# A gated linear attention with two feed-forward stages on one core: split weights kept in DRAM, solver steps and the chain placed anew

## The chip, the cores and the metric

The kernel runs on 1 of the 8 cores of a Trainium2 chip. The metric is the device time of the program in microseconds (us), the median of the timed runs. The profile is of one execution more, with its own time.

## The reference, cut to what matters

```
# attention: B, H, S, D = 4, 8, 768, 48; delta rule, one state (D x D) for each batch and head
k_n = k / (norm(k) + 1e-6)
for t in range(S):
    y[t] = q[t] @ state
    state = state + beta[t] * outer(k_n[t], v[t] - k_n[t] @ state)
x = y, as 3072 tokens x 384
x = (x @ w_a) * (x @ w_b) @ w_out                  # d_ff 1536
h = x @ w_in                                       # d_ff 2048
out = (max(h, 0) + alpha * min(h, 0)) @ w_out2
```

All is float32. The kernel keeps the precision of the big products by splitting every operand into a high and a low part in the 32-bit matmul format fp32r (hi, and lo = raw - hi) and summing three matmuls: hi*hi, hi*lo, lo*hi.

## The kernel before, in words

**Tiles and units.** The 768 steps are cut into 12 chunks of 64 (T) steps, and two chunks (a pair) of all four batches make one tile of 512 tokens, six tiles (NP) in all. In a tile the two feed-forward stages run as 68 units (NU, `tile_units`, L197). A unit is one 128 x 384 piece of a weight against the tile: A f and BB f (x times w_a and w_b, 9 matmuls of 512 columns each), O f (times w_out, 9 of 512), H f (times w_in, 9 of 512) and Y f (times the second w_out, 12 of 384). The order is A0, BB0, then A f, BB f, O f-1 for f = 1 to 11 (so BB f is unit 3f, O f is unit 3f+4), O11 as unit 35 (`last_o`), H0, H1, then H f, Y f-2, and Y14, Y15. The number m = 68 i + n names unit n of tile i.

**The order of all work** is one list, `seq`, written by hand (L169 to L262). Every engine walks through this list and does its own part of each entry, in order. Beside each unit of tile i, the lists of `beside(i + 1)` (L211) hang the attention work of the next pair: transposes (TR) and Gram products (GG, DG), a solver that inverts a 32 x 32 triangular block for every head and half on VectorE (IN, 34 steps ROW 1 to 34, XT; `solver`, L724), and the chain (H1, H2, H3, H4, HS, HY for each of the two chunks, L160), in which TensorE makes small matmuls and ScalarE or VectorE evacuates them before the next stage can start. VS (L937, GpSimd) scales v by the key norms. Before the first tile a prologue does all this for pair 0 and parts of pair 1, with idle time of TensorE filled by throw-away matmuls F (L450).

Where `beside` puts things before: ROW 1 to 14 four per unit from unit 11, ROW 15 to 18 at units 15 to 18, ROW 19 to 34 one per unit at units 19 to 34; XT and VS of the first chunk at unit 35, VS of the second at 36; H1 at 35, then H2 at 38 and one chain stage at every unit up to HY of the second chunk at 48; the reload of x (XL) at 50; norms of the next pair at 51 to 54. Loads of k, q for the pair after (LTK, LTQ) stand at units 8 to 15, LK at 17 and 19.

**Weights.** There is a ring of 9 slots (RG). WL n (L343, SyncE's queue) waits until the unit that used the slot 9 units ago is done and loads 192 KB into `w_raw`: O and Y as rows of 1536 B, A, BB and H as rows of 512 B. WS n stands 4 units (RS) ahead of unit n: ScalarE casts `w_raw` to `w_hi` (L669) and GpSimd subtracts to `w_lo` (L952), which lies in the memory of `w_raw`. TensorE waits for `lo_ok` before each unit. So each of the 408 pieces is loaded and split anew in each of the six tiles.

**Within a unit.** For BB f, VectorE makes g_sb from e_sb and the bank (L895), ScalarE casts it to g_hi (L691), VectorE subtracts to g_lo (L906, entry GL, which stands behind all that `beside` hangs on that unit), and O f needs g_lo. For H f, ScalarE makes e_sb and f_sb (L687, L688), VectorE g_sb (L900), then g_hi and g_lo as above. After O11 the three banks are evacuated to m_hi, m_lo (M, L698, L911) for H0.

In the chain, H1 is evacuated by VectorE, which waits for VS of its chunk:

```
                    dve.wait_ge(*is_full(*st))
                    dve.wait_ge(v_ok, c + 1)
                    dve.tensor_tensor(r_sb[:, hf], v_raw[:, c % 2, units(hf), :], chained(hf), ALU.subtract
```

and H2 on TensorE waits for XT:

```
                        pe.wait_ge(solve, NSOL * p + NSOL)
```

Of the kernel before, what the change touches and what calls it, by code (L numbers as in the profile page):

```python
# [8 lines left out]
F32 = mybir.dt.float32  # L9
# [5 lines left out]
def build(nc, q, k, v, beta, wa, wb, wo, win, wout, alpha, out):  # L15
# [25 lines left out]
    assert 2 * T == P and 2 * U == SB and TILE == 512  # L41

    ctx = ExitStack()
    with ctx:
# [21 lines left out]
        with ExitStack() as whole:  # L66
            w_raw = sb("w_raw", [P, RG, DM], F32, whole)
            x_raw = sb("x_raw", [P, KC, TILE], F32, whole)
            g_sb = sb("g_sb", [P, GR, TILE], F32, whole)
        w_lo = sb("w_lo", [P, RG, DM], F32R)  # L70
        x_lo = sb("x_lo", [P, KC, TILE], F32R)
        g_lo = sb("g_lo", [P, GR, TILE], F32R)
        w_hi = sb("w_hi", [P, RG, DM], F32R)
        x_hi = sb("x_hi", [P, KC, TILE], F32R)
# [95 lines left out]
        seq += [("LV", 0), ("LV", 1), ("B",)] + [("F", 0)] * 4 + flat(norms(0))  # L170
        for hf in range(2):
            seq += [("TRK", 2 * hf)] + [("F", 0)] * 3 + [("TRK", 2 * hf + 1)] + [("F", 0)] * 2
            seq += [("GK", 0, hf), ("GK", 1, hf), ("DG0", hf)]
        seq += [("IN", 0)]
        for b in range(B):
            seq += [("LTK", 1, b), ("LTQ", 1, b)]
        seq += [("LK", 1, 0), ("LK", 1, 1)] + [("WL", n) for n in range(RG)] + [("VS", 0), ("VS", 1)]
        for n in range(1, ROWS + 1):
# [3 lines left out]
                    21: [("GQ", 1, 0)], 22: [("GQ", 1, 1)]}.get(n, [])  # L182
        seq += [("XT", 0), ("F", ROWS), ("F", ROWS)]
        beside0 = {(0, "H2"): [("PT", 0), ("PT", 1), ("SQ", 2)], (0, "H3"): [("PT", 2), ("PT", 3), ("KS", 2), ("SQ", 3)],
                   (0, "H4"): [("KS", 3), ("KN", 1)], (0, "HS"): [("KI", 1), ("LV", 2)], (0, "HY"): [("XL", 0, 0, T)],
                   (1, "H1"): [("WS", 0)], (1, "H2"): [("WS", 1)], (1, "H3"): [("WS", 2)], (1, "H4"): [("WS", 3)]}

        for kind in ("H2", "H3", "H4", "HS", "HY"):
            seq += both(kind, 0) + [("F", 0)] + beside0.get((0, kind), [])
        for kind in ("H1", "H2", "H3", "H4", "HY", "HS"):  # L190
# [20 lines left out]
        def beside(p):  # L211
            at = [[] for _ in range(NU)]
            if p >= NP:
                return at
            if p > 1:
                for g in range(8):
                    at[g // 2].append(("TR", p, g))
                for g in range(4):
                    at[4 + g // 2].append(("GG", 2 * p, g))
                    at[6 + g // 2].append(("GG", 2 * p + 1, g))  # L220
                for j in range(2):
                    at[6 + j].append(("DG", 2 * p, j))
                    at[8 + j].append(("DG", 2 * p + 1, j))

            s = 10
            at[s].append(("IN", p))
            for n in range(1, ROWS + 1):
                at[s + ((n + 3) // 4 if n <= R8 else 4 + n - R8 if n <= R16 else 8 + n - R16)].append(("ROW", p, n))
            at[s + 8 + ROWS - R16 + 1] += [("XT", p), ("VS", 2 * p)]
            at[s + 8 + ROWS - R16 + 2].append(("VS", 2 * p + 1))  # L230

            s += 8 + ROWS - R16 + 3
            for n, st in enumerate(chain(2 * p) + chain(2 * p + 1)):
                m = s + n // 2 if n >= 2 else last_o
                at[m].append(st)
                if p + 1 < NP and st[0] == "H2" and st[2] == 0:
                    at[m].append(("LV", st[1] + 2))
            s += len(chain(0)) + 1
            at[s].append(("XL", p, 0, P))
            if p + 1 < NP:  # L240
                for b in range(B):
                    at[8 + 2 * b].append(("LTK", p + 1, b))
                    at[9 + 2 * b].append(("LTQ", p + 1, b))
                for j in range(2):
                    at[17 + 2 * j].append(("LK", p + 1, j))
                for j, part in enumerate(norms(p + 1)):
                    at[s + 1 + j] += part
            return at

        for i in range(NP):  # L250
            for n, (st, extra) in enumerate(zip(tile_units(i), beside(i + 1))):
                m = NU * i + n
                seq += [st] + [("WL", m + RG)] * (m + RG < NU * NP) + [("WS", m + RS)] * (m + RS < NU * NP)
                if st[0] == "O" and st[2] == NF1 - 1:
                    seq += [("M", i, kc) for kc in range(KC)]
                seq += extra
                if st[0] in ("BB", "H"):
                    seq.append(("GL", i, st[2] + NF1 * (st[0] == "H")))
# [49 lines left out]
        def _(sp):  # L308
            for st in seq:
# [33 lines left out]
                elif kind == "WL":  # L343
# [38 lines left out]
        def _(pe):  # L382
            def three(dst, lhs_hi, lhs_lo, rhs_hi, rhs_lo, start, stop):
                pe.matmul(dst, lhs_hi, rhs_hi, start=start, stop=False)  # L384
                pe.matmul(dst, lhs_hi, rhs_lo, start=False, stop=False)  # L385
                return pe.matmul(dst, lhs_lo, rhs_hi, start=False, stop=stop)  # L386

            def in_bank(*st):
# [6 lines left out]
            for st in seq:  # L395
# [126 lines left out]
                elif kind in ("A", "BB"):  # L522
# [18 lines left out]
                elif kind == "O":  # L541
# [16 lines left out]
                elif kind == "H":  # L558
# [417 lines left out]
```

## Time and profile before

| what | us |
|---|---|
| median of 3 timed runs (1168.53 to 1175.56) | 1168.88 |
| the profiled execution, whole time | 1172.99 |
| its span, first to last instruction | 1171.3 |

In the views, PE is TensorE (matmuls), PEld its weight loads, DVE VectorE, ACT ScalarE, POOL GpSimd, SP SyncE with its DMA queue. In brackets behind a row of the order of time stands how long the engine sat idle before it, and what released it. Matmuls are pipelined: one 128x512 matmul is shown with 0.39 us but the next starts 0.227 us after it, so durations of units are read from the start of one to the start of the next. Granted clock 1.00 is the upper of TensorE's two levels (2.4 GHz), 0.50 the lower (1.2 GHz).

The view of busy time by stretch has these columns: the stretch (us from the span's start) and its length, then busy us (and number of instructions) of PE, PEld, DVE, ACT and POOL, the granted clock, the mean busy share of the 16 DMA engines and the GB/s that they moved.

### The profile page before, as it was taken

To read this page: it belongs to the slowest core of one execution; us is meant where nothing else is said; L and a number is where in the kernel's file an instruction comes from. 1 tells how busy PE (TensorE), PEld (TensorE's weight loads), DVE (VectorE), ACT (ScalarE), POOL (GpSimd) and SP (SyncE) were. 2 spreads that over 40 slices of the span, in tenths; PEclk is the share of its full clock that TensorE was granted. 3 is DMA by queue.
4 is the path that set the end of the run, shared out by engine and by line. 5 is a ranking of instruction groups with operands and counts; after the bars stand their busy time and mean duration, and the time that the engine had idled before them with its cause. 6 is when DMAs were issued, how large, how long until landed. Compare 5 with 4: busy or idle time off the path is not lost.

```text
span 1171.3 us, 24961 instructions
## 1 busy us (share of the span) xinstructions
PE 1122.2 (96%) x10390; PEld 948.6 (81%) x10390; DVE 585.2 (50%) x849; ACT 530.4 (45%) x1054; POOL 477.7 (41%) x432
## 2 busy tenths in 40 slices
PE   5899999999998999999999999899999999999998
PEld 3587877898886889887789888689888778988898
DVE  5834774334577334387424377533348733422333
ACT  2134343365434356543436554345644334644564
POOL 0012562245364225255224446423536522555453
PEclk9889998999999999999899999899999989999999
DMA  9721732233452234272224354223323212443331
GB/s 118 150 43 50 180 90 62 64 108 108 116 135 81 57 89 122 69 168 82 63 59 121 99 136 122 68 63 102 115 63 101 75 43 61 117 122 98 92 95 61
DMA packets 235919, 110.26 MB, mean 94 GB/s; under 512 B 111376, under 2 KB 235808, under 8 KB 235808
## 3 DMA queue, kind: packets, MB, share of 16 engines
q1 hardware_dynamic: 235776, 108.66, 36.3%
q8 instruction: 83, 1.36, 0.5%
q14 instruction: 28, 0.23, 0.1%
q0 software_dynamic: 32, 0.01, 0.0%
HBM read 99.20 MB, written 4.72 MB: 89 GB/s over the span
## 4 chain that ended last, share of the span: by engine, by line
PE 87%; DVE 7%; ACT 3%; issue 1%; DMA 0%; SPq 0%; POOL 0%; DVEq 0%; POOLq 0%
PE bank L384 24%; PE bank L385 23%; PE bank L386 23%; PE bank L447 3%; PE bank L463 2%; PE bank L484 2%; PE bank L520 2%; PE bank L519 2%; PE bank L497 2%; PE bank L487 2%; DVE g_sb L900 2%; PE bank L404 1%; DVE x_lo L884 1%; DVE prod L782 1%; PE bank L481 1%
## 5 line engine op out<-in xcount | busy, mean ns | idle before, releaser
L952 POOL TENSOR_TENSOR w_lo<-w_raw,w_hi 128x384 fp32r<-128x384 f32 x408 | 457.6, 1135 | 637.2 <-ACT w_hi L669 636.3
L691 ACT CAST g_hi<-g_sb 128x512 fp32r<-128x512 f32 x168 | 104.2, 620 | 242.9 <-DVE g_sb L895 144.8
L669 ACT CAST w_hi<-w_raw 128x384 fp32r<-128x384 f32 x408 | 196.9, 511 | 0.3
L900 DVE SCALAR_TENSOR_TENSOR g_sb<-f_sb,neg_alpha,e_sb 128x512 f32<-128x512 f32 x96 | 82.2, 857 | 210.7 <-ACT f_sb L688 205.4
L384 PE MATMUL bank<-x_hi,w_hi 128*128 128x512 f32 x432 | 172.0, 398 | 3.0 <-DVE x_lo L884 2.6
L385 PE MATMUL bank<-x_lo,w_hi 128*128 128x512 f32 x432 | 169.1, 391 | 0.0
L386 PE MATMUL bank<-x_hi,w_lo 128*128 128x512 f32 x432 | 168.8, 391 | 0.0
L906 DVE TENSOR_TENSOR g_lo<-g_sb,g_hi 128x512 fp32r<-128x512 f32 x168 | 120.5, 717 | 74.3 <-ACT g_hi L691 72.7
L687 ACT ACTIVATE e_sb<-bank 128x512 f32<-128x512 f32 x96 | 57.2, 596 | 170.5 <-PE bank L386 170.5
L384 PE MATMUL bank<-w_hi,g_hi 128*128 128x384 f32 x384 | 132.1, 344 | 0.0
L386 PE MATMUL bank<-w_hi,g_lo 128*128 128x384 f32 x384 | 129.2, 337 | 0.0
L385 PE MATMUL bank<-w_lo,g_hi 128*128 128x384 f32 x384 | 128.8, 335 | 0.0
L895 DVE TENSOR_TENSOR g_sb<-e_sb,bank 128x512 f32<-128x512 f32 x72 | 49.4, 686 | 154.5 <-PE bank L386 154.5
L384 PE MATMUL bank<-m_hi,w_hi 128*128 128x512 f32 x288 | 119.0, 413 | 0.1
L385 PE MATMUL bank<-m_lo,w_hi 128*128 128x512 f32 x288 | 116.4, 404 | 0.0
L386 PE MATMUL bank<-m_hi,w_lo 128*128 128x512 f32 x288 | 116.1, 403 | 0.0
L384 PEld LDWEIGHTS bank<-x_hi,w_hi 128*128 128x128 f32 x432 | 81.4, 188 | 23.1 <-DVE x_lo L884 4.9
L384 PE MATMUL bank<-g_hi,w_hi 128*128 128x512 f32 x216 | 87.5, 405 | 11.5 <-DVE g_lo L906 11.5
L680 ACT COPY e_sb<-bank 128x512 f32<-128x512 f32 x72 | 42.3, 587 | 124.0 <-PE bank L386 123.6
L386 PEld LDWEIGHTS bank<-x_hi,w_lo 128*128 128x128 f32 x432 | 81.5, 189 | 17.2
L385 PEld LDWEIGHTS bank<-x_lo,w_hi 128*128 128x128 f32 x432 | 81.6, 189 | 16.1
L385 PE MATMUL bank<-g_lo,w_hi 128*128 128x512 f32 x216 | 87.0, 403 | 0.0
(105 smaller groups left out, 1714.0 us busy)
## 6 DMA issues: line engine op xcount, KB each, us to landing
w_raw<-in_moe_w_out_dram SPq DMA_DIRECT2D x168, 192.0 KB, 2.4
w_raw<-in_moe_w_in_dram SPq DMA_DIRECT2D x96, 192.0 KB, 2.4
w_raw<-in_moe_w_a_dram SPq DMA_DIRECT2D x72, 192.0 KB, 2.5
w_raw<-in_moe_w_b_dram SPq DMA_DIRECT2D x72, 192.0 KB, 2.6
k_raw<-in_k_dram SPq DMA_DIRECT2D x24, 192.0 KB, 4.1
k_tok<-in_k_dram SPq DMA_DIRECT2D x24, 192.0 KB, 3.4
q_tok<-in_q_dram SPq DMA_DIRECT2D x24, 192.0 KB, 3.4
v_raw<-in_v_dram SPq DMA_DIRECT2D x24, 192.0 KB, 3.9
```

What stands on the lines that cost most here:

```text
L384: pe.matmul(dst, lhs_hi, rhs_hi, start=start, stop=False)
L385: pe.matmul(dst, lhs_hi, rhs_lo, start=False, stop=False)
L386: return pe.matmul(dst, lhs_lo, rhs_hi, start=False, stop=stop)
L447: mm = pe.matmul(bk[h, 2 * T * j:2 * T * (j + 1)], kq[rows, w, e, 0], kq[rows, w, e].rearrange("p i t -> p (i t)"), start=True, stop=True)
L669: act.copy(w_hi[:, n % RG], w_raw[:, n % RG]).then_inc(hi_ok, 1)
L680: act.copy(e_sb[:, f % 2], h_bank[0][:, :]).then_inc(e_ok, 1)
L687: act.activation(e_sb[:, f % 2], h_bank[f % 2][:, :], ACT.Relu).then_inc(e_ok, 1)
L691: act.copy(g_hi[:, j % GR], g_sb[:, j % GR]).then_inc(gh_ok, 1)
L895: dve.tensor_tensor(g_sb[:, j % GR], e_sb[:, f % 2], h_bank[1][:, :], ALU.mult).then_inc(g_ok, 1)
L900: dve.scalar_tensor_tensor(g_sb[:, j % GR], f_sb[:, f % 2], neg_alpha[:, f:f + 1], e_sb[:, f % 2], ALU.mult, ALU.add).then_inc(g_ok, 1)
L906: dve.tensor_tensor(g_lo[:, s], g_sb[:, s], g_hi[:, s].bitcast(F32), ALU.subtract).then_inc(gl_ok, 1)
L952: pool.tensor_tensor(w_lo[:, r], w_raw[:, r], w_hi[:, r].bitcast(F32), ALU.subtract).then_inc(lo_ok, 1)
```

## The change

1. A DRAM scratch tensor of 68 x 128 x 768 floats is added. `w_hi` and `w_lo` of a slot now lie side by side in one tensor `w_two`. In the first tile each unit's split pair, 384 KB in rows of 3072 B, is stored to it (new entry WT, on SyncE's queue). From the second tile on, WL loads that pair straight into `w_two`; WS isn't done there, and TensorE waits for the load itself (`weights`).
2. The solver's steps stand at other units: ROW 1 to 14 seven per unit at 11 and 12, ROW 15 to 18 at 13 to 16, ROW 19 to 34 at 17 to 28 by the list `r16`; XT and the first VS at 29, the second VS at 31.
3. The chain stands at units 28, 30, 31, 32, 33, 34 (first chunk) and 35, 37, 39, 41, 43, 45 (second chunk); XL at 46, the norms at 47 to 50.
4. In the prologue, the second half's transposes stand ahead of the first half's block copies, four more F follow XT, and two F instead of one stand behind each of the five chain stages of chunk 0.

```diff
+    split = nc.dram_tensor("split_scratch", (NU, P, 2 * DM), F32).ap()
...
-            w_raw = sb("w_raw", [P, RG, DM], F32, whole)
+            w_ring = sb("w_ring", [P, RG, 2, DM], F32, whole)
...
-        w_lo = sb("w_lo", [P, RG, DM], F32R)
+        w_raw = w_ring[:, :, 1]
+        w_two = sb("w_two", [P, RG, 2, DM], F32R)
+        w_hi, w_lo = w_two[:, :, 0], w_two[:, :, 1]
...
-        for hf in range(2):
-            seq += [("TRK", 2 * hf)] + [("F", 0)] * 3 + [("TRK", 2 * hf + 1)] + [("F", 0)] * 2
-            seq += [("GK", 0, hf), ("GK", 1, hf), ("DG0", hf)]
-        seq += [("IN", 0)]
+        seq += [("TRK", 0)] + [("F", 0)] * 3 + [("TRK", 1)] + [("F", 0)] * 2 + [("GK", 0, 0), ("GK", 1, 0)]
+        seq += [("TRK", 2)] + [("F", 0)] * 3 + [("TRK", 3)] + [("DG0", 0), ("GK", 0, 1), ("GK", 1, 1), ("DG0", 1), ("IN", 0)]
...
-        seq += [("XT", 0), ("F", ROWS), ("F", ROWS)]
+        seq += [("XT", 0)] + [("F", ROWS)] * 6
...
-                   (1, "H1"): [("WS", 0)], (1, "H2"): [("WS", 1)], (1, "H3"): [("WS", 2)], (1, "H4"): [("WS", 3)]}
+                   (1, "H1"): [("WS", 0)], (1, "H2"): [("WS", 1)], (1, "H3"): [("WS", 2)], (1, "H4"): [("WS", 3)],
+                   (1, "HY"): [("WT", 0), ("WT", 1)], (1, "HS"): [("WT", 2)]}
...
-            seq += both(kind, 0) + [("F", 0)] + beside0.get((0, kind), [])
+            seq += both(kind, 0) + [("F", 0)] * 2 + beside0.get((0, kind), [])
...
             for n in range(1, ROWS + 1):
-                at[s + ((n + 3) // 4 if n <= R8 else 4 + n - R8 if n <= R16 else 8 + n - R16)].append(("ROW", p, n))
-            at[s + 8 + ROWS - R16 + 1] += [("XT", p), ("VS", 2 * p)]
-            at[s + 8 + ROWS - R16 + 2].append(("VS", 2 * p + 1))
-
-            s += 8 + ROWS - R16 + 3
+                r16 = (7, 8, 9, 9, 10, 10, 11, 11, 11, 12, 13, 14, 15, 16, 17, 18)
+                at[s + ((n + 6) // 7 if n <= R8 else 2 + n - R8 if n <= R16 else r16[n - R16 - 1])].append(("ROW", p, n))
+            at[s + 19] += [("XT", p), ("VS", 2 * p)]
+            at[s + 21].append(("VS", 2 * p + 1))
+
+            stages = (28, 30, 31, 32, 33, 34, last_o, last_o + 2, last_o + 4, last_o + 6, last_o + 8, last_o + 10)
             for n, st in enumerate(chain(2 * p) + chain(2 * p + 1)):
-                m = s + n // 2 if n >= 2 else last_o
+                m = stages[n // 2]
...
-            s += len(chain(0)) + 1
+            s = stages[-1]
+            s += 1
             at[s].append(("XL", p, 0, P))
...
-                seq += [st] + [("WL", m + RG)] * (m + RG < NU * NP) + [("WS", m + RS)] * (m + RS < NU * NP)
+                seq += [st] + [("WL", m + RG)] * (m + RG < NU * NP) + [("WS", m + RS)] * (m + RS < NU)
+                seq += [("WT", m + RS - 1)] * (m + RS - 1 < NU)
...
                     if n >= RG:
                         sp.wait_ge(unit_ok, n - RG + 1)
-                    if which in ("O", "Y"):
+                        if n - RG < NU:
+
+                            sp.wait_ge(w_st[n % RG], 16 * ((n - RG) // RG + 1))
+                    if n >= NU:
+                        sp.dma_start(w_two[:, n % RG].bitcast(F32).rearrange("p i c -> p (i c)"), split[u]).then_inc(w_ld[n % RG], 16)
+                    elif which in ("O", "Y"):
...
+                elif kind == "WT":
+                    n = st[1]
+                    sp.wait_ge(lo_ok, n + 1)
+                    sp.dma_start(split[n], w_two[:, n % RG].bitcast(F32).rearrange("p i c -> p (i c)")).then_inc(w_st[n % RG], 16)
...
+            def weights(n):
+                if n < NU:
+                    pe.wait_ge(lo_ok, n + 1)
+                else:
+                    pe.wait_ge(w_ld[n % RG], 16 * (n // RG) + 16)
...
-                    pe.wait_ge(lo_ok, n + 1)
+                    weights(n)
```

The last replacement is made in all four kinds of unit (A and BB, O, H, Y).

## Rows read from the trace of the kernel before

**Rows 1.** Busy time by stretch: prologue, tiles 0, 1, 2, last tile.

```profile
0.00:97.70 97.70, 77.75 (x1310) 56.31 (x1310) 58.44 (x105) 29.27 (x56) 9.69 (x18) 0.90 0.58 94
97.70:275.50 177.80, 172.68 (x1556) 147.81 (x1556) 90.69 (x124) 79.46 (x160) 78.32 (x69) 0.96 0.38 98
275.50:462.70 187.20, 182.09 (x1716) 155.11 (x1716) 98.51 (x143) 88.06 (x175) 80.46 (x71) 0.98 0.37 98
462.70:651.00 188.30, 183.17 (x1716) 156.52 (x1716) 98.50 (x143) 88.06 (x175) 80.45 (x71) 0.97 0.37 97
...
1026.50:1171.30 144.80, 141.25 (x660) 121.22 (x660) 45.04 (x64) 70.97 (x142) 68.17 (x66) 1.00 0.31 93
```

**Rows 2.** Waits of PE, whole span: us in total, times, longest.

```profile
PE bank L484 <- ACT w_sb L652: 14.2, 5, 2.9
PE bank L384 <- DVE g_lo L906: 11.5, 6, 2.2
```

**Rows 3.** PE in order of time, tile 1: start, us, engine, line, operation.

```profile
340.88 0.39 PE L384 MATMUL bank<-x_hi,w_hi 128*128 128x512 f32 x1
...
342.92 0.39 PE L384 MATMUL bank<-x_hi,w_hi 128*128 128x512 f32 x1
...
361.63 0.49 PE L384 MATMUL bank<-g_hi,w_hi 128*128 128x512 f32 x1 [2.23 <-DVE g_lo L906]
...
365.44 2.07 PE L463 MATMUL bank<-state,kq 48*64 48x48 f32 x64
...
380.46 1.55 PE L484 MATMUL bank<-w_sb,gs 32*32 32x48 f32 x64 [2.80 <-ACT w_sb L652]
...
385.68 1.60 PE L487 MATMUL bank<-r_sb,xt 32*32 32x48 f32 x64
...
407.55 1.55 PE L484 MATMUL bank<-w_sb,gs 32*32 32x48 f32 x64
...
411.26 1.55 PE L487 MATMUL bank<-r_sb,xt 32*32 32x48 f32 x64
```

**Rows 4.** DVE in order of time, tile 1, around the two stalls.

```profile
358.10 2.02 DVE L782 TENSOR_TENSOR prod<-inv,mid 128x1024 f32<-128x1024 f32 x1
...
366.77 2.14 DVE L789 STREAM_TRANSPOSE xt<-inv 128x1024 f32<-128x1024 f32 x1
368.80 0.98 DVE L857 TENSOR_TENSOR r_sb<-v_raw,bank 128x384 f32<-128x384 f32 x2
...
373.99 2.05 DVE L900 SCALAR_TENSOR_TENSOR g_sb<-f_sb,neg_alpha,e_sb 128x512 f32<-128x512 f32 x1 [0.80 <-PE bank L386]
...
378.21 0.75 DVE L900 SCALAR_TENSOR_TENSOR g_sb<-f_sb,neg_alpha,e_sb 128x512 f32<-128x512 f32 x1 [0.80 <-ACT f_sb L688]
```

**Rows 5.** POOL and ACT in order of time, tile 1, second stall.

```profile
374.02 1.47 POOL L945 TENSOR_TENSOR v_raw<-v_raw,knorm 128x768 f32<-128x768 f32 x1
...
379.94 0.85 ACT L652 COPY w_sb<-bank 128x384 f32<-128x384 f32 x2
```

**Rows 6.** ACT and POOL behind an A unit, tile 0.

```profile
118.01 0.59 ACT L680 COPY e_sb<-bank 128x512 f32<-128x512 f32 x1 [1.84 <-PE bank L386]
118.50 0.52 ACT L669 CAST w_hi<-w_raw 128x384 fp32r<-128x384 f32 x1
...
119.09 1.01 POOL L952 TENSOR_TENSOR w_lo<-w_raw,w_hi 128x384 fp32r<-128x384 f32 x1 [1.18 <-ACT w_hi L669]
```

**Rows 7.** Busy time by stretch: loads of k and q, of weights.

```profile
12.50:15.00 2.50, 2.50 (x48) 1.60 (x48) 1.01 (x5) 1.01 (x2) 0.00 (x0) 1.00 1.51 164
...
50.00:52.50 2.50, 1.71 (x6) 0.42 (x4) 2.47 (x2) 0.00 (x0) 1.51 (x2) 0.77 1.05 313
```

**Rows 8.** DMA issues: count, KB each, median us to landing.

```profile
w_raw<-in_moe_w_out_dram SPq DMA_DIRECT2D x168, 192.0 KB, 2.4
```

**Rows 9.** PE in the prologue: H3 of chunk 0 and of chunk 1.

```profile
56.19 2.77 PE L484 MATMUL bank<-w_sb,gs 32*32 32x48 f32 x64
...
71.92 1.55 PE L484 MATMUL bank<-w_sb,gs 32*32 32x48 f32 x64
```

More of the change, by code:

```diff
@@ L66, in build @@
         with ExitStack() as whole:
-            w_raw = sb("w_raw", [P, RG, DM], F32, whole)
+            w_ring = sb("w_ring", [P, RG, 2, DM], F32, whole)
             x_raw = sb("x_raw", [P, KC, TILE], F32, whole)
             g_sb = sb("g_sb", [P, GR, TILE], F32, whole)
-        w_lo = sb("w_lo", [P, RG, DM], F32R)
+        w_raw = w_ring[:, :, 1]
+        w_two = sb("w_two", [P, RG, 2, DM], F32R)
+        w_hi, w_lo = w_two[:, :, 0], w_two[:, :, 1]
         x_lo = sb("x_lo", [P, KC, TILE], F32R)
         g_lo = sb("g_lo", [P, GR, TILE], F32R)
-        w_hi = sb("w_hi", [P, RG, DM], F32R)
         x_hi = sb("x_hi", [P, KC, TILE], F32R)
@@ L123, in build @@
         dg_ok, dgv_ok, solve = sem("dg_ok"), sem("dgv_ok"), sem("solve")
-        w_ld = [sem(f"w_ld{n}") for n in range(RG)]
+        w_ld, w_st = [sem(f"w_ld{n}") for n in range(RG)], [sem(f"w_st{n}") for n in range(RG)]
         hi_ok, lo_ok, unit_ok = sem("hi_ok"), sem("lo_ok"), sem("unit_ok")
@@ L547, in _ @@
                         pe.wait_ge(od_ok, 2 * i)
-                    pe.wait_ge(lo_ok, n + 1)
+                    weights(n)
                     pe.wait_ge(gl_ok, NF * i + f + 1)
@@ L566, in _ @@
                         pe.wait_ge(f_ok, NF2 * i + f - 1)
-                    pe.wait_ge(lo_ok, n + 1)
+                    weights(n)
                     for kc in range(KC):
@@ L578, in _ @@
                     r = n % RG
-                    pe.wait_ge(lo_ok, n + 1)
+                    weights(n)
                     pe.wait_ge(gl_ok, NF * i + NF1 + f + 1)
```

## Prediction, made before the changed kernel was run

> **What bounds the kernel now.** I read the busy times by stretch first, then TensorE's waits, then the order of time of each engine around the waits. TensorE is busy in 97% of a middle tile (182.1 of 187.2 us), VectorE, ScalarE and GpSimd in about half of it [rows 1]. So only what stops TensorE or slows it counts. Its pace elsewhere is fixed: a unit of 9 matmuls takes 342.92 - 340.88 = 2.04 us [rows 3], and the last tile, with no attention beside it, takes 144.8 us for its 68 units [rows 1].
>
> Two waits make up nearly all idle time of TensorE behind the prologue, each once in each of the five tiles that carry attention: g_lo 2.2 us before O11, and w_sb 2.8 us before H3 [rows 2]. After each, TensorE is slow for a few us more: O11 takes 365.44 - 361.63 = 3.81 us, where a unit with a chain stage behind it takes some 2.2; H3 and the unit behind it take 385.68 - 380.46 = 5.22, while the same pair one chunk later takes 411.26 - 407.55 = 3.71 [rows 3]. A stall thus costs its idle time and a slow stretch: 2.23 + 1.6 = 3.8 us, and 2.80 + 1.5 = 4.3 us, 8.1 us a tile. Every second tile is 1.1 us longer with the same busy instructions (188.3 against 187.2) [rows 1], which I read as a longer slow stretch: 9.2 us there.
>
> Why they arise: the first, because VectorE runs a solver product of 2.02 us between g_sb and g_lo of BB11 [rows 4], and O11 follows BB11 by one unit only. The second, because g_sb of an H unit takes 2.05 us instead of 0.75 [rows 4], from the same moment on which GpSimd runs VS (374.02, 1.47 us) [rows 5]; ScalarE gets to w_sb only behind that unit's and the next one's casts.
>
> **The change part by part, against the profiled execution (1172.99 us; its span 1171.3; it lies 4.1 us above the median of the runs).**
>
> *Solver and chain moved, tiles 1 to 4.* No solver step stands at BB11 (unit 33) any more; HY stands at unit 34 between it and O11, 2 times about 1.9 us of matmuls, so g_lo has 5.8 us, of which it needs some 3 (g_sb, the HS evacuation, g_lo). The first stall goes whole. H3 of chunk 2 stands at unit 31 behind H2 at 30: on ScalarE g_hi and two w_sb copies (0.85) [rows 5] against one unit of 2.04; it fits. H3 of the next chunk has two units behind H2, and VS is gone from there: GpSimd has nothing else to do from tile 1 on, so it does VS for the next pair as soon as the norms are there, near unit 50, where H f and Y f have five units between them. The second stall goes whole. What is late next? XT must be there at H2, behind unit 30. Counted from the end of BB9 (unit 27): VectorE does g_sb, a solver step of 1.9, g_lo, one of 1.2 (4.4 us), two H1 evacuations (0.98) and XT (2.14) [rows 4]: 7.6 us. TensorE does O8, H1, A10, BB10: 2.1 + 2.0 + 2.2 + 2.1 = 8.4. It fits by 0.8 us. M at unit 35 keeps H1 as its cover. Sum: 8.1 x 2 + 9.2 x 2 = -34.6 us.
>
> *The same in tile 0.* Its two stalls go, -9.2. But here the solution of pair 1 needs VS, and GpSimd's queue has WS of unit 33 ahead of it, whose cast stands on ScalarE behind the copy of A10 (unit 29). VectorE's H1 at unit 28 waits for this VS and holds XT behind it, and TensorE's H2 waits for XT. From the end of A10: e_sb and cast 1.0, w_lo to 2.1 [rows 6], VS 1.47 [rows 5] to 3.6, two evacuations to 4.6, XT to 6.7 [rows 4]. TensorE has only BB10 (2.1): idle 4.6 us, and by the two stalls above a slow stretch of 1.5 to 4, taken as 2.5. +7.1. Tiles 1 to 4 have no WS, so this is tile 0's alone. Net -2.1.
>
> *Weights loaded split.* ScalarE loses 340 casts of 0.51, GpSimd 340 subtractions of about 1 us [rows 5, 6]: neither ends a wait other than those two, so nothing more comes back; the rest was cover. In tiles 1 to 5 SyncE issues one load a unit as before, 384 KB instead of 192, 9 units ahead (18 us; a load of today lands in 2.4 [rows 8]) and no longer 4 units ahead of a cast. The wait on w_st asks for a store issued three units before, also nothing. No row shows 3 KB rows moving. Rates that rows do show: 313 GB/s while weights are loaded, 164 GB/s while k and q come in 192 B rows [rows 7]. So 384 KB take 1.26 or 2.4 us; were the packets the whole cost, a third of a 192 KB load's 0.63, 0.2 us. I take 1.26, the row with the longest runs. At 1.26 tiles 1 to 5 have room (1.26 of 2.04 us).
>
> *Stores in tile 0.* From unit 0 to 19: 20 loads x 0.63 + 20 stores x 1.26 + 12 loads of k and q x 1.2 = 52.2 us of DMA beside 42.6 us of TensorE: 9.6 us behind. A load is issued 5 units (10.2) ahead of its cast and lands in 2.4, so 7.8 are free; ScalarE and then TensorE wait 1.8 us. With 0.2 us a store: nothing; with 2.4: see below. I put +1. SyncE itself issues at most three DMAs of 0.4 us a unit; behind a WT that waits for lo_ok it holds the next WL, four units early, so nothing.
> By the Trainium skill's "SBUF — State Buffer", section "A bandwidth-pool intuition that's wrong (but worth ruling out)", a core gets about 358 GB/s of HBM; a store would then take an estimated 1.10 us, the queue be 6.4 us behind, and this term 0 instead of 1. The 313 GB/s of the row lie below that figure; no row reaches down to decide it.
>
> *Prologue (97.7 us).* The reordered copies take one of two ScalarE block copies off the path to the solver, about -1. Four more F fall into XT's 2 us. Five more F cost 0.3 to 0.54 each (+2), and if they bring the upper clock back sooner, each stage of chunk 0 wins up to 2.77 - 1.55 = 1.2 us [rows 9] (-5 at most). I take -1 in all, between +2 and -5. Loads of the first weights have over 20 us.
>
> *Against the removal of GpSimd's work:* with subtractions still running in tile 0, VectorE keeps being held there as in rows 4. In "SBUF — State Buffer", section "SBUF: two separate sides", the Trainium skill calls the port that VectorE and GpSimd share an exclusive lock for the whole instruction. Row and rule agree on the 2.05 us; by it the 0.8 us of room before XT would go only in tile 0, where that wait is lost already.
>
> Sum: -34.6 - 2.1 + 1 - 1 = -36.7. Profiled 1136.3 us; on the scale of the median 1168.9 - 36.7 = **1132 us**.
>
> **The rivals.**
> 1. *DMA sets tile 0* (chance 0.13). For it: stores double what the queue carries and k, q, v come on top. Against: rows 7's 313 GB/s were reached with a third of the run length. At 1.6 us a store the early part is 52.2 + 6.8 = 59 us, 16.4 behind, 8.6 us of stall instead of 1, with its slow stretch +9: 1141. Sign: queue share near 1 over tile 0.
> 2. *The moved solver is late in every tile* (0.10): 0.8 us of room before XT turns into a wait, by queueing I can't see. About 1 us idle and 2 slow, four tiles: +12, 1144. The change then does two thirds of what it says.
> 3. *Tile 0 doesn't stall at v* (0.12), or the F bring the clock back: -7, 1125. Against it stands the order of the queues alone.
> 4. *Slower than before* (0.03): 3 KB rows move no faster than the 192 B rows, 2.4 us for 384 KB. Then 68 loads take 163 us a tile, plus 16 attention loads x 1.2 = 19: 182 against a clean tile of 179 (187.2 - 8.1): +3 x 4; the last tile 163 instead of 142, +21; tile 0 68 x 3.03 + 19 = 225 instead of 176, +49. 1132 + 82 = 1214. It decides from about 2.35 us a load in tiles 1 to 4, 2.1 in the last one.
>
> **How the numbers follow.** Forecast 0.62 (own range 1126 to 1139, from the prologue's ends and the slow stretch), rivals 0.13, 0.10, 0.12, 0.03. The range takes in rivals 1 to 3 and the few us by which executions differ: 1119 to 1146. A measurement of this kernel tells 1% (12 us) from no change: faster by more in all cases but the fourth and unknown ones, 0.94; within 1% 0.03; slower 0.03.
>
> **What would show it.** Right: a middle tile of 179 us in the busy times by stretch, the waits for g_lo and w_sb gone from TensorE's list in tiles 0 to 4, GpSimd busy only in the first quarter of the span, DMA at 130 to 160 GB/s from tile 1 on. In tile 0 one new wait of 4 to 5 us before H2 at unit 30, released by XT. Wrong: a TensorE wait on a split_scratch load, VectorE's XT ending after BB10 in tiles 1 to 4, a tile 0 longer than 180 us.

## The result and the profile after

The changed kernel takes 1132.04 us (median of 4 runs, 1130.89 to 1133.91) against 1170.03 us before (4 runs); the ratio is 0.967, with a 95% interval of 0.963 to 0.970. The forecast was 1132 us. The profiled execution took 1133.91 us with a span of 1132.2, 39.1 us less than before.

Busy time by stretch of the changed kernel, in the columns of [rows 1]: prologue, tiles 0, 1, 2 and the last one, cut at the first matmul of each.

```profile
0.00:95.23 95.23, 75.11 (x1318) 52.88 (x1318) 58.25 (x105) 29.19 (x56) 9.68 (x18) 0.96 0.63 109
95.23:273.34 178.11, 173.12 (x1557) 147.80 (x1557) 90.73 (x124) 78.01 (x157) 80.14 (x68) 0.96 0.76 248
273.34:452.03 178.69, 178.69 (x1717) 153.48 (x1717) 89.27 (x143) 60.16 (x107) 3.79 (x2) 1.00 0.62 178
452.03:630.60 178.57, 178.57 (x1718) 153.38 (x1718) 88.63 (x142) 60.17 (x107) 3.79 (x2) 1.00 0.61 178
987.73:1132.20 144.47, 141.00 (x661) 121.15 (x660) 43.03 (x62) 44.78 (x78) 0.00 (x0) 1.00 0.56 176
```

In tiles 1 and 2 TensorE's busy time now equals the stretch, at a granted clock of 1.00, the upper level (2.4 GHz); before it was 182 of 187 us at 0.98 [rows 1]. Each of tiles 1 to 4 is 178.6 us long, the alternation of 187 and 188 is gone. GpSimd has two instructions a tile left, the DMA moves 178 GB/s instead of 98. Tile 0 is as long as before, 178.1 us against 177.8. The prologue is 2.5 us shorter, the last tile 0.3. Executions of the kernel before differ by 7 us (1168.53 to 1175.56), and the profiled one lies above their median, so the difference of the profiles (39.1) is a little larger than that of the medians (38.0).

TensorE's waits over the whole span, to be held against [rows 2] (us in total, times, longest; line numbers are those of the changed kernel: L502 is H2, L399 a big matmul):

```profile
PE bank L502 <- DVE xt L810: 4.7, 1, 4.7
...
PE bank L399 <- DVE x_lo L905: 2.6, 1, 2.6
...
PE bank L399 <- DVE g_lo L927: 0.6, 2, 0.3
```

The w_sb wait of 14.2 us is gone, that for g_lo fell from 11.5 to 0.6, and one new wait has come, in tile 0. VectorE in order of time around it, then GpSimd and TensorE:

```profile
158.99 1.47 DVE L927 TENSOR_TENSOR g_lo<-g_sb,g_hi 128x512 fp32r<-128x512 f32 x1
160.38 1.21 DVE L807 TENSOR_REDUCE inv<-prod 128x64 f32<-128x1024 f32 x1
165.97 1.02 DVE L878 TENSOR_TENSOR r_sb<-v_raw,bank 128x384 f32<-128x384 f32 x2 [4.37 <-POOL v_raw L966]
166.90 2.00 DVE L810 STREAM_TRANSPOSE xt<-inv 128x1024 f32<-128x1024 f32 x1
```

```profile
163.42 1.01 POOL L973 TENSOR_TENSOR w_two<-w_ring,w_two 128x384 fp32r<-128x384 f32 x1 [2.08 <-ACT w_two L690]
164.39 1.47 POOL L966 TENSOR_TENSOR v_raw<-v_raw,knorm 128x768 f32<-128x768 f32 x1
```

```profile
169.01 2.36 PE L502 MATMUL bank<-r_sb,xt 32*32 32x48 f32 x64 [4.66 <-DVE xt L810]
```

This is the chain of waits that was forecast: the subtraction behind the cast of unit 33, then VS, then the H1 evacuations, which were free to run 4.37 us earlier, then XT, then H2.

One engine's rows show something else, VectorE's product of 128x768 in tile 0 and, with nothing on GpSimd, in tile 1:

```profile
153.12 2.37 DVE L803 TENSOR_TENSOR prod<-inv,mid 128x768 f32<-128x768 f32 x1
...
338.88 1.61 DVE L803 TENSOR_TENSOR prod<-inv,mid 128x768 f32<-128x768 f32 x1
```

### The profile page after: what moved, and what is told of

The parts are those of the page before. It is cut to its first block, busy times and chain, and to the rows that moved or that the text cites. A ratio compares the mean times of both kernels' runs of the same rounds, so it can differ in the third digit from the quotient of the medians.

```text
span 1132.2 us, 24435 instructions
## 1 busy us (share of the span) xinstructions
PE 1103.6 (97%) x10397; PEld 935.4 (83%) x10397; DVE 544.2 (48%) x849; ACT 390.9 (35%) x714; POOL 101.2 (9%) x92
## 4 chain that ended last, share of the span: by engine, by line
PE 91%; DVE 6%; issue 1%; ACT 1%; POOL 0%; DMA 0%; SPq 0%; DVEq 0%; POOLq 0%
PE bank L399 25%; PE bank L401 24%; PE bank L400 24%; PE bank L468 3%; PE bank L541 2%; PE bank L540 2%; PE bank L484 2%; PE bank L518 2%; PE bank L502 2%; PE bank L505 2%; PE bank L425 1%; PE bank L508 1%; PE bank L475 1%; DVE prod L803 1%; DVE prod L796 1%
## 5 line engine op out<-in xcount | busy, mean ns | idle before, releaser
L399 PE MATMUL bank<-x_hi,w_two 128*128 128x512 f32 x432 | 173.8, 402 | 2.7 <-DVE x_lo L905 2.6
L400 PE MATMUL bank<-x_lo,w_two 128*128 128x512 f32 x432 | 169.7, 393 | 0.0
L401 PE MATMUL bank<-x_hi,w_two 128*128 128x512 f32 x432 | 169.4, 392 | 0.0
L401 PE MATMUL bank<-w_two,g_lo 128*128 128x384 f32 x384 | 129.4, 337 | 0.0
L399 PE MATMUL bank<-w_two,g_hi 128*128 128x384 f32 x384 | 129.3, 337 | 0.0
L400 PE MATMUL bank<-w_two,g_hi 128*128 128x384 f32 x384 | 128.9, 336 | 0.0
L399 PE MATMUL bank<-m_hi,w_two 128*128 128x512 f32 x288 | 115.6, 401 | 0.1
L401 PE MATMUL bank<-m_hi,w_two 128*128 128x512 f32 x288 | 113.5, 394 | 0.0
L400 PE MATMUL bank<-m_lo,w_two 128*128 128x512 f32 x288 | 113.3, 393 | 0.0
L399 PEld LDWEIGHTS bank<-x_hi,w_two 128*128 128x128 f32 x432 | 81.7, 189 | 22.1 <-DVE x_lo L905 3.3
L401 PEld LDWEIGHTS bank<-x_hi,w_two 128*128 128x128 f32 x432 | 81.8, 189 | 17.5
L400 PEld LDWEIGHTS bank<-x_lo,w_two 128*128 128x128 f32 x432 | 81.9, 190 | 15.6
L399 PE MATMUL bank<-g_hi,w_two 128*128 128x512 f32 x216 | 87.6, 406 | 0.6 <-DVE g_lo L927 0.6
L400 PE MATMUL bank<-g_lo,w_two 128*128 128x512 f32 x216 | 85.0, 394 | 0.0
L401 PE MATMUL bank<-g_hi,w_two 128*128 128x512 f32 x216 | 84.8, 393 | 0.0
```

## The experiments

All were timed against the kernel before on the same chip. They come from three chips, so between experiments the ratios say more than the medians. "Tile 1" is the second tile, from its first matmul to the next one's.

### The parts by themselves

**The split weights alone** (e1_weights): the changed kernel with solver, chain and prologue as before.

```diff
...
-            at[s + 19] += [("XT", p), ("VS", 2 * p)]
-            at[s + 21].append(("VS", 2 * p + 1))
...
+            at[s + 8 + ROWS - R16 + 1] += [("XT", p), ("VS", 2 * p)]
+            at[s + 8 + ROWS - R16 + 2].append(("VS", 2 * p + 1))
...
-            stages = (28, 30, 31, 32, 33, 34, last_o, last_o + 2, last_o + 4, last_o + 6, last_o + 8, last_o + 10)
+            s += 8 + ROWS - R16 + 3
...
-                m = stages[n // 2]
+                m = s + n // 2 if n >= 2 else last_o
...
```

> The split weights alone (part 1), with the solver, the chain and the prologue as before. Theory: the w_sb wait goes with GpSimd's and ScalarE's work, the g_lo wait stays, since the solver's product of 1.9 us still stands between g_sb and g_lo of BB11; it is shorter by the 0.75 us for which g_lo itself was held. Tiles 1 to 4 then take 178.6 + 1.5 idle + 1.6 slow = 181.7 us, tile 0 177.8, the span 97.7 + 177.8 + 4 x 181.7 + 144.5 = 1147 us. Rival, the placing does it all: both waits stay, tiles of 187 to 188, span 1171.

Measured: 1142.81 us, ratio 0.977 (0.974 to 0.980), span 1143.1. Tile 1 takes 180.4 us. TensorE's waits in it:

```profile
362.30 0.47 PE L399 MATMUL bank<-g_hi,w_two 128*128 128x512 f32 x1 [1.45 <-DVE g_lo L927]
...
377.03 1.55 PE L505 MATMUL bank<-w_sb,gs 32*32 32x48 f32 x64 [0.30 <-ACT w_sb L673]
```

The w_sb wait is down to 0.30 us with the chain left where it was, the g_lo wait to 1.45, about the 1.5 that were expected. What was not: no slow stretch follows it, and from H3 to H4 it takes 3.72 us. In tile 0, where GpSimd still subtracts, both waits stay (2.2 and 2.9 us). Of the 36.6 us that tiles 1 to 4 gained together, this part alone gives 29 (four tiles of 180.4 against 751.0 us before).

**The new places alone** (e2_places): parts 2 and 3 on the kernel before.

```diff
-                at[s + ((n + 3) // 4 if n <= R8 else 4 + n - R8 if n <= R16 else 8 + n - R16)].append(("ROW", p, n))
-            at[s + 8 + ROWS - R16 + 1] += [("XT", p), ("VS", 2 * p)]
...
+                at[s + ((n + 6) // 7 if n <= R8 else 2 + n - R8 if n <= R16 else r16[n - R16 - 1])].append(("ROW", p, n))
+            at[s + 19] += [("XT", p), ("VS", 2 * p)]
...
```

> The new places of solver and chain alone (parts 2 and 3) on the kernel before. Theory: GpSimd still has a subtraction per unit in every tile, so VS of the first chunk is late in all five tiles as it was in tile 0 of the changed kernel (4.7 us idle and 3.3 slow): tiles of 178 (tile 0) and 178.6 + 8 = 186.6, span 97.7 + 178 + 4 x 186.6 + 144.7 = 1167 us, no gain worth the name. Rival, the two parts add up: the placing alone removes both waits, span 1135.

Measured: 1178.66 us, ratio 1.008 (1.005 to 1.011): slower than before by more than its interval. TensorE's waits:

```profile
PE bank L483 <- DVE xt L791: 23.2, 5, 4.7
PE bank L386 <- DVE g_lo L908: 6.6, 10, 0.9
```

The wait of tile 0 stands in all five tiles, 4.65 us each, and tiles 1 to 4 take 188.6 to 189.9 us. The mechanism was that of the theory; its price was 2 to 3 us a tile too low, for two short g_lo waits a tile and the slow stretches. So with VS at units 29 and 31 the placing is worth something only where GpSimd doesn't subtract: 180.4 - 178.6 = 1.8 us a tile on top of the split weights. Without them it costs 1.4 to 1.7 us a tile (188.6, 189.7, 188.9 and 189.9 against 187.2, 188.3, 187.2 and 188.3).

**The F of the prologue** (e3_old_f).

```diff
-        seq += [("XT", 0)] + [("F", ROWS)] * 6
+        seq += [("XT", 0), ("F", ROWS), ("F", ROWS)]
...
-            seq += both(kind, 0) + [("F", 0)] * 2 + beside0.get((0, kind), [])
+            seq += both(kind, 0) + [("F", 0)] + beside0.get((0, kind), [])
```

> The changed kernel with the F matmuls of before in the prologue (two behind XT, one behind each stage of chunk 0), the reordered copies kept. Theory: the F hold the upper clock, so without them chunk 0 runs at the lower one (stages of 2.7 us) and A0 starts 2.5 us later; the first unit wins 1.2 back: span 1133.5. Rival, the reordered copies won the 2.5 us: span unchanged, 1132.2.

Measured: 1132.88 us, ratio 0.969 (0.966 to 0.971), span 1131.0. The F do hold the clock: H2, H3 and H4 of chunk 0, first in the changed kernel, then without the added F.

```profile
54.01 1.55 PE L502 MATMUL bank<-r_sb,xt 32*32 32x48 f32 x64
56.03 1.55 PE L505 MATMUL bank<-w_sb,gs 32*32 32x48 f32 x64
58.05 1.55 PE L508 MATMUL bank<-r_sb,xt 32*32 32x48 f32 x64
```

```profile
52.18 1.55 PE L502 MATMUL bank<-r_sb,xt 32*32 32x48 f32 x64 [1.01 <-POOL r_sb L966]
53.98 2.24 PE L505 MATMUL bank<-w_sb,gs 32*32 32x48 f32 x64
56.69 2.77 PE L508 MATMUL bank<-r_sb,xt 32*32 32x48 f32 x64
```

But A0 starts at 96.11 against 95.23 us, and by the end of tile 0 the kernel without them is 1.1 us ahead in its profile, because its tile 0 takes 176.1 us and not 178.1. H2 of chunk 0 starts 54.01 - 52.18 = 1.8 us later with them, of which 0.9 had arisen before any added F (the second pair of GK starts at 19.32 against 18.46 us). What the F are worth in all lies below what these runs tell apart: in the profiles of three kernels with the same prologue (the changed one, e4 and e7 below) tile 0 starts at 95.23, 93.93 and 94.11 us. The six profiles with the old prologue (the kernel before, e1, e2, e8, e9, e10) have it at 96.4 to 98.8, 97.8 in the mean, so the new order and the F together are worth some 3 us.

### What made the two waits

**VS alone** (e8_before_vs), on the kernel before.

```diff
-            at[s + 8 + ROWS - R16 + 1] += [("XT", p), ("VS", 2 * p)]
-            at[s + 8 + ROWS - R16 + 2].append(("VS", 2 * p + 1))
+            at[s + 8 + ROWS - R16 + 1].append(("XT", p))
+            at[s + 12].append(("VS", 2 * p))
+            at[s + 13].append(("VS", 2 * p + 1))
```

> The kernel before with nothing moved but VS, from units 35 and 36 to 22 and 23. Theory: g_sb of H1 takes 0.75 us again, so w_sb comes 1.3 us earlier and the wait before H3 falls from 2.8 to 1.5 us in each of five tiles; the g_lo wait stays: span 1171.3 - 6.5 = 1165. Rival, the port isn't what holds g_sb: 1171.

Measured: 1155.06 us, ratio 0.989 (0.986 to 0.992), span 1153.3: 18 us less in the profiles and 13.6 in the medians, instead of 6.5. TensorE at H3 and H4 of tile 1:

```profile
375.19 1.55 PE L485 MATMUL bank<-w_sb,gs 32*32 32x48 f32 x64 [1.52 <-ACT w_sb L653]
...
378.93 1.55 PE L488 MATMUL bank<-r_sb,xt 32*32 32x48 f32 x64
```

The wait is the expected 1.5 us. But from H3 to H4 it is now 3.74 us, not 5.22 [rows 3]: the slow stretch is gone with the last part of the stall, and with it the longer tile in every second place (184.2 to 184.3 us each). A wait of 1.5 us costs 1.5 here, one of 2.8 costs 4.3 and more.

**g_lo ahead of the solver's steps** (e9_gl_first), on the kernel before.

```diff
-                seq += extra
                 if st[0] in ("BB", "H"):
                     seq.append(("GL", i, st[2] + NF1 * (st[0] == "H")))
+                seq += extra
```

> The kernel before with one entry moved in the list: g_lo of a BB or H unit stands ahead of what hangs beside the unit, not behind it. Theory: the solver's product no longer lies between g_sb and g_lo of BB11, so the g_lo wait falls from 2.2 to the bare chain's 0.3 us and its slow stretch goes, 3.8 us in each of five tiles; the w_sb wait stays: span 1171.3 - 19 = 1152. Rival: VectorE now stands idle 0.7 us for g_hi in each BB unit, its solver steps slip past H2's need of XT, and half of it is lost: 1161.

Measured: 1168.13 us, ratio 0.997 (0.996 to 0.999), span 1166.2. Both theories fall. The same two places in tile 1:

```profile
356.28 0.47 PE L384 MATMUL bank<-g_hi,w_hi 128*128 128x512 f32 x1 [0.31 <-DVE g_lo L906]
...
374.20 2.77 PE L484 MATMUL bank<-w_sb,gs 32*32 32x48 f32 x64 [3.21 <-ACT w_sb L652]
...
380.97 1.55 PE L487 MATMUL bank<-r_sb,xt 32*32 32x48 f32 x64
```

The first wait is gone, as expected, and the tile is as long as ever (187.6 us; tiles 2 to 4 take 187.7, 187.8 and 186.9, tile 0 175.2 instead of 177.9). The second wait grew from 2.80 to 3.21, H3 itself now runs at the lower clock (2.77 us), and from H3 to H4 it takes 380.97 - 374.20 = 6.77 us where it took 5.22 [rows 3]. Unit by unit against tile 1 of the kernel before: O10 and O11 with H1 win 1.9 and 1.3 us; the unit in which the w_sb wait and H3 stand loses 1.6, units 20 to 22, where VectorE now stands idle for g_hi, 0.55, and five further places 0.2 to 0.4 each. So a stall of 2.2 us was taken away and its gain given back behind it, half of it in the other stall. Why that one grew by 0.4 us can be read from VectorE:

```profile
361.80 2.22 DVE L789 STREAM_TRANSPOSE xt<-inv 128x1024 f32<-128x1024 f32 x1
363.92 0.96 DVE L857 TENSOR_TENSOR r_sb<-v_raw,bank 128x384 f32<-128x384 f32 x2
364.81 0.73 DVE L900 SCALAR_TENSOR_TENSOR g_sb<-f_sb,neg_alpha,e_sb 128x512 f32<-128x512 f32 x1
```

TensorE now comes earlier to H0, but XT and the H1 evacuations don't, so g_sb of H0 has to wait behind them (before, VectorE stood idle for 1.27 us ahead of it). ScalarE waits 1.31 us for this g_sb instead of 0.92, and w_sb stands behind it in ScalarE's queue.

**Both** (e10_gl_vs): the edit above, and VS at units 4 and 5.

```diff
-            at[s + 8 + ROWS - R16 + 1] += [("XT", p), ("VS", 2 * p)]
-            at[s + 8 + ROWS - R16 + 2].append(("VS", 2 * p + 1))
+            at[s + 8 + ROWS - R16 + 1].append(("XT", p))
+            at[4].append(("VS", 2 * p))
+            at[5].append(("VS", 2 * p + 1))
```

> The kernel before with two moves in the list only: g_lo ahead of what hangs beside its unit, and VS at units 4 and 5. No DRAM scratch, all weights split anew in each tile, solver and chain where they were. Theory: the two waits are all that the change removes, so this comes near it: tiles of 184.2 - 3.8 = 180.4, span 1153.3 - 19 = 1134, against 1132.2 of the changed kernel. Rival: the w_sb wait comes back to its 2.8 us because VectorE's queue shifts: 1145 or more.

Measured: 1156.9 us, ratio 0.987 (0.984 to 0.991), span 1155.3; no better than VS alone. The w_sb wait stays at 9.6 us in five tiles, 1.9 each, again 0.4 us more than without g_lo ahead (1.5 in e8):

```profile
PE bank L485 <- ACT w_sb L653: 9.6, 5, 1.9
```

and four of the five are followed by a slow stretch: from H3 to H4 it takes 5.3 us in tiles 1, 3 and 4, 6.5 in tile 2, but 3.75, the full pace, in tile 0. With VS away, what stands ahead of w_sb on ScalarE is three H units' worth of e, f and g_hi and the casts of the weights between them; e1 took those casts and the subtractions away, and the wait was 0.3. That the casts and not GpSimd's subtractions are the larger share of this last piece was not tried apart.

### Tile 0

**VS earlier in the changed kernel** (e4_vs_early): XT stays at unit 29, VS goes to 22 and 23.

```diff
-            at[s + 19] += [("XT", p), ("VS", 2 * p)]
-            at[s + 21].append(("VS", 2 * p + 1))
+            at[s + 19].append(("XT", p))
+            at[s + 12].append(("VS", 2 * p))
+            at[s + 13].append(("VS", 2 * p + 1))
```

> The changed kernel with VS at units 22 and 23 instead of 29 and 31. Theory: tile 0's only long wait (4.66 us before H2, 3.3 us slow behind it) goes, tile 0 takes 170 us, span 1124.3. Rival 1, tile 0 is held by the DMA queues (share 1.04 in units 18 to 32): the wait goes but others come, span 1129 or more. Rival 2, VectorE, busy 27.6 of 28 us there, is what is late: VS moved into that stretch holds it longer, g_lo waits grow, span 1127.

Measured: 1124.53 us, ratio 0.960 (0.957 to 0.963), span 1122.2. Tile 0 takes 169.4 us and the 4.66 us wait is gone. Of the 8.7 us that the tile is shorter than in the changed kernel's profile, VS gives 5.9: 7.8 are won at H2 and the unit behind it, 1.9 lost around a new wait. The other 2.8 are not its work. They come from the first two units, which stand behind the same wait of 2.65 us for x_lo and run at another granted clock, 0.57 in the changed kernel and 1.00 in e4 (busy time by stretch, one line each):

```profile
95.23:102.24 7.01, 7.01 (x18) 5.55 (x19) 0.00 (x0) 1.80 (x4) 1.01 (x1) 0.57 0.21 75
```

```profile
93.93:98.14 4.21, 4.21 (x18) 3.49 (x19) 0.00 (x0) 1.81 (x4) 0.63 (x1) 1.00 0.11 29
```

The new wait, 1.54 us, stands at O8, in a stretch where GpSimd stood behind VS and VectorE's solver:

```profile
153.44 0.50 PE L400 MATMUL bank<-g_hi,w_two 128*128 128x512 f32 x1 [1.54 <-POOL w_two L974]
```

**Stores doubled** (e7_store_twice), timed once.

```diff
+    again = nc.dram_tensor("again_scratch", (NU, P, 2 * DM), F32).ap()
...
-                            sp.wait_ge(w_st[n % RG], 16 * ((n - RG) // RG + 1))
+                            sp.wait_ge(w_st[n % RG], 32 * ((n - RG) // RG + 1))
...
-                    sp.dma_start(split[n], w_two[:, n % RG].bitcast(F32).rearrange("p i c -> p (i c)")).then_inc(w_st[n % RG], 16)
+                    for to in (split, again):
+                        sp.dma_start(to[n], w_two[:, n % RG].bitcast(F32).rearrange("p i c -> p (i c)")).then_inc(w_st[n % RG], 16)
```

> The changed kernel with each split pair stored twice, to two scratch tensors. It prices a store of 384 KB where nothing but the DMA can be late. Theory, 1.26 us a store at the 313 GB/s of the kernel before: tile 0 has 68 x (0.63 + 2.52) + 19 = 233 us of DMA and becomes as long, 55 us more: span 1187. Rival, 3 KB rows store at 400 GB/s or more (1.0 us): 68 x 2.6 + 19 = 196, span 1150.

Measured: 1151.41 us, span 1149.7, 17.5 us more than the changed kernel, near the rival's number. Busy time by stretch in tile 0, units 18 to about 30 and the ones behind, and 20 us of the latter:

```profile
134.00:162.00 28.00, 23.23 (x110) 17.21 (x110) 17.02 (x22) 6.75 (x13) 8.76 (x9) 1.00 1.06 345
162.00:200.00 38.00, 28.19 (x449) 22.92 (x447) 14.68 (x17) 9.22 (x19) 13.81 (x12) 0.82 1.00 359
164.00:184.00 20.00, 10.60 (x87) 8.55 (x88) 9.30 (x9) 5.70 (x12) 8.63 (x8) 0.72 1.04 388
```

With the queues full the DMA moves 345 and 359 GB/s in the two stretches, so 384 KB (393,216 bytes) cost by estimate 393.2 / 359 = 1.10 us and not 1.26. The Trainium skill gives about 358 GB/s of HBM for a core ("SBUF — State Buffer", section "A bandwidth-pool intuition that's wrong (but worth ruling out)"). The 38 us agree with that figure, but it is no upper bound here: the 20 us inside them show 388 GB/s, which would be 1.01 us for 384 KB. Nor is the rival's price of 1.0 us borne out by the span: over all of tile 0 (195.8 us, where it said 196) the DMA moves 333 GB/s and not 400. TensorE then waits 7.3 us in ten pieces for w_lo, 3.8 us once for g_lo and 8.4 us for XT. In the changed kernel the first of these stretches moves 315 GB/s at a share of 1.03, and no wait of TensorE ends in a load.

### A version that beats both

**XS ahead of the last two GG** (e5_xs_early).

```diff
-        seq += [("TR", 1, g) for g in range(8)] + [("GG", 2, g) for g in range(4)] + [("GG", 3, g) for g in range(4)]
-        seq += [("XS", 0, kc) for kc in range(KC)] + [("DG", c, j) for c in (2, 3) for j in range(2)]
+        seq += [("TR", 1, g) for g in range(8)] + [("GG", 2, g) for g in range(4)] + [("GG", 3, 0), ("GG", 3, 1)]
+        seq += [("XS", 0, kc) for kc in range(KC)] + [("GG", 3, 2), ("GG", 3, 3)] + [("DG", c, j) for c in (2, 3) for j in range(2)]
```

> The changed kernel with the three XS of tile 0 ahead of the last two GG of the prologue, in the list of all work. Theory: x_lo is ready when TensorE ends its last GG, so the 2.65 us before A0 and the slow stretch behind it (1.96 + 0.97) go: span 1132.2 - 5.6 = 1126.6. Rival, VectorE's evacuations, pushed behind x_lo, hold TensorE's last GG instead: no more than 1 us won, span 1131.

Measured: 1129.52 us, ratio 0.964 (0.961 to 0.967), span 1126.9. The wait before A0 falls from 2.65 to 0.62 us. In the profile it is worth 5.3 us where 5.6 were expected, in the medians 2.5, and the interval of the ratio overlaps that of the changed kernel (0.963 to 0.970). The profile flatters it: the first two units, which took 7.0 us in the changed kernel's profile, take 4.5 here, and e4 has them at 4.2 with the wait still there. The 2.0 us of wait are the part that is sure.

**Both moves** (e6_both): the diffs of e4 and e5 together, with VS at 22 and 23.

> Both moves together. Theory: they add up, span 1132.2 - 7.9 - 5.6 = 1118.7. Rival: an earlier start of tile 0 by 5.6 us brings its DMA queue behind (the loads of k, q stand at units 8 to 19), part of it is lost: 1121 or more.

Measured: 1122.07 us, ratio 0.958 (0.954 to 0.961), span 1120.3: 10 us less than the changed kernel in the medians, with the O8 wait of 1.5 us still there. That the DMA takes the rest isn't seen in any wait.

**VS at units 4 and 5** (e11_best), where VectorE has no solver step, and XS moved as in e5:

```diff
-            at[s + 19] += [("XT", p), ("VS", 2 * p)]
-            at[s + 21].append(("VS", 2 * p + 1))
+            at[s + 19].append(("XT", p))
+            at[4].append(("VS", 2 * p))
+            at[5].append(("VS", 2 * p + 1))
```

> The changed kernel with VS at units 4 and 5, where VectorE has nothing to do, instead of 22 and 23, and XS of tile 0 ahead of the last two GG. Theory: the 1.54 us wait for w_lo at unit 28, which VS at 22 and 23 brought by holding GpSimd's queue, goes with its slow stretch of 1.7: span 1120.3 - 3.2 = 1117. Rival: that wait comes from the subtractions held by VectorE's solver steps, with or without VS: 1120.

Measured: 1120.48 us, ratio 0.957 (0.954 to 0.959), span 1118.9, the lowest of all, though its interval overlaps that of e6. Its prologue, tile 0 and tile 1:

```profile
0.00:91.62 91.62, 73.76 (x1317) 52.14 (x1317) 56.98 (x102) 27.52 (x53) 9.68 (x18) 0.96 0.66 113
91.62:260.06 168.44, 167.54 (x1557) 143.29 (x1557) 92.32 (x128) 79.67 (x159) 80.33 (x68) 1.00 0.80 262
260.06:438.73 178.67, 178.67 (x1717) 153.48 (x1717) 89.30 (x143) 60.16 (x107) 3.79 (x2) 1.00 0.64 179
```

The O8 wait is gone, so it was VS in GpSimd's queue that had brought it; tile 0 won 1.4 us over e6, half of what was expected. The whole of tile 0 runs at the upper clock with the stores in it.

The same trace bears on what the split weights are worth. Tile 0 still splits all 68 pieces and stores them, tile 1 loads them ready; from unit 8 on both have nearly the same list (ahead of it, tile 1 holds transposes and Gram products that the prologue did for tile 0). Unit 8 to the end of tile 0, then of tile 1:

```profile
108.59:260.06 151.47, 150.72 (x1486) 129.72 (x1484) 87.09 (x119) 70.53 (x142) 71.20 (x60) 1.00 0.82 267
288.49:438.73 150.24, 150.24 (x1487) 130.07 (x1485) 79.09 (x122) 49.80 (x88) 3.79 (x2) 1.00 0.66 182
```

With the new places and VS this early, splitting costs 1.2 us a tile, by estimate 5 us in tiles 1 to 4. So most of what the DRAM scratch brings to the change may be had by VS alone. The kernel before with the new places and VS at units 4 and 5, which would show it, was not run.

**g_lo first, on top** (e12_best_gl): e11 with the edit of e9.

```diff
-                seq += extra
                 if st[0] in ("BB", "H"):
                     seq.append(("GL", i, st[2] + NF1 * (st[0] == "H")))
+                seq += extra
```

> The kernel of the run above with g_lo ahead of what hangs beside its unit as well. Theory: nothing in tiles 1 to 4, where no wait is left; in tile 0 the 0.28 us wait for g_lo at unit 25 and the longer unit ahead of it go, 0.7 us: span 1116.5. Rival: VectorE, full in units 18 to 28 of tile 0, loses 0.7 us at each BB unit and XT comes late: 1120 or more.

Measured: 1127.59 us, ratio 0.963 (0.960 to 0.966), 7 us slower than e11. TensorE's waits:

```profile
PE bank L503 <- DVE xt L811: 2.5, 1, 2.5
PE bank L400 <- DVE g_sb L917: 1.4, 2, 0.9
```

The rival held: VectorE stands idle for g_hi in each BB unit, and in tile 0 it has no such time to give. Tiles 1 to 4 lose 0.2 us each.

## Why the prediction was right, and where it was not

**The sum.** Forecast -36.7 us; measured -39.1 in the profiled executions and -38.0 in the medians. By stretch:

| stretch | forecast | measured |
|---|---|---|
| prologue | -1 | -2.5 |
| tile 0 | -2.1 + 1 | +0.3 |
| tiles 1 to 4 | -34.6 | -36.6 |
| last tile | 0 | -0.3 |

That the median of 1132.04 us meets the 1132 to a tenth is luck: the parts are off by -1.5, +1.4, -2.0 and -0.3 us and partly cancel, and the kernel before alone has medians from 1168.6 to 1173.2 us on the chips of the runs.

**Tiles 1 to 4.** 179 us were forecast, 178.6 measured, with no wait left. The step that gave it was right: a stall costs its idle time and the slow stretch behind it. So was the reading that every second tile has a longer one: from H3 to H4 it takes 5.2 us in tiles 1 and 3 of the kernel before and 6.5 in tiles 2 and 4, behind the same wait of 2.8 us. The room before XT was put at 0.8 us. XT ends at 348.21 + 2.22 = 350.4 and H2 starts at 351.16, so it is 0.7:

```profile
348.21 2.22 DVE L810 STREAM_TRANSPOSE xt<-inv 128x1024 f32<-128x1024 f32 x1
```

```profile
351.16 1.55 PE L502 MATMUL bank<-r_sb,xt 32*32 32x48 f32 x64
```

**What the sum hid.** The prediction booked the -34.6 under "solver and chain moved" and wrote of the split weights that "nothing more comes back". By the runs it is the other way round as long as VS stands where the change puts it. The weights alone give 1168.6 to 1142.8 us, the new places alone cost 10 us, and both (with the prologue) give 38. The prediction had the link in hand, as it noted that VS is late wherever GpSimd still subtracts, and used it for tile 0 only; it did not ask what each part would be worth without the other. Nor is the DRAM scratch the only way to free VS: moved to earlier units it is on time beside all subtractions (tile 0 of e4 and e11).

**The second wait.** Named was VS, which holds g_sb, with ScalarE's casts behind. VS is 1.3 of its 2.8 us (e8: 1.5 left), the casts and subtractions nearly all the rest (e1: 0.3 left). In "SBUF — State Buffer", section "SBUF: two separate sides", the Trainium skill has VectorE and GpSimd lock their shared port for a whole instruction. The runs agree in that g_sb takes 2.05 us beside VS [rows 4] and the product above 2.37 us beside subtractions, 1.61 without.

**Tile 0.** The 4.6 us of idle time were right to 0.1 (4.66). The slow stretch was mis-sized: H2 takes 2.29 us instead of 1.48, the O unit behind it 4.14 instead of 2.3, H3 1.88 instead of 1.48, 3.1 us in all where 2.5 stood. Short waits for g_lo (0.6 us in two) were not in the sum. A slower first unit (4.00 us instead of 2.83) wasn't either, but it belongs to this one execution and not to the change (e4 has 2.17 behind the same wait). Without it tile 0 would have gained some 0.9 us of the 1.1 that were forecast, and not lost 0.3.

**Stores.** The +1 us was 0: no wait of TensorE ends in a load or store, and a store costs less than the row it was priced by (by estimate 1.0 to 1.1 us under full queues, from e7). The reading that the early stretch is close to full was right, a share of 1.03 from 134 to 166 us.

**Prologue.** -1 in all, with ends of +2 and -5; it is -2.5 in this profile and -3.4 in the mean of three profiles against six, of which e3 can't give a share to the F beyond 1 us.

**The rivals.** DMA setting tile 0 needed 1.6 us a store, and the estimate is 1.1 at most: out. A late solver in every tile: out, by 0.7 us. A stall in tile 0 that doesn't come: out. Slower than before: out for the change, but its sign came true for parts 2 and 3 alone.

## What to carry to other kernels

Price each part of a change with the other parts absent: here one part was worth 26 us, another cost 10 us by itself, and together they gave 38, since the second, with VS where it stood, needs an engine that the first sets free. Before an item is moved in a hand-written order, look at the queue that feeds it (VS behind the subtractions on GpSimd) as well as at the engine that waits for it. A wait that is taken away in front of another one may only make the next longer (e9). Before a slow stretch behind a wait is booked to a change, look for it in a second execution with the same order of work there.

## What the runs showed of the hardware that was not expected

- What follows a wait of TensorE isn't set by the length of the wait alone. Behind 1.45 us (e1, four tiles) and 1.5 to 1.6 us (e8, five tiles) the next units ran at full pace. Behind 1.9 us (e10) the way from H3 to H4 took 3.75 us once, 5.3 three times and 6.5 once; behind 2.8 us in the kernel before 5.2 and 6.5 by turns. The wait of 2.65 us before A0 was followed by 7.0 us for two units in one execution (granted clock 0.57) and by 4.2 in another (1.00). What decides is not shown. Going from 2.8 to 1.5 us was worth 13.6 us in the medians (VS moved by itself, e8), where the idle time alone made 6.5.
- VectorE's own work in tile 0 takes longer beside GpSimd: a product of 128x768 2.37 us instead of 1.61, g_lo 1.47 instead of 0.69, so that VectorE was full (27.6 of 28 us, from 132 to 160 us) by holding and not by work.
- The share of the DMA engines is no measure of the room left: 178 GB/s show 0.62 in tile 1, 315 GB/s show 1.03 (134 to 162 us), and doubled stores still raised the rate to 388 GB/s at 1.04 (164 to 184 us of e7).
